# Local attention in ten blocks of 57 queries on a 64x64-split array, in place of five blocks of 120 queries

## The chip, the cores and the metric

One core of one Trainium2 chip. The metric is the device time of one execution in microseconds, the median of three runs. All inputs and outputs are float32.

## The reference

Attention over 4 x 8 heads of 576 positions and 64 columns has two parts: one over positions averaged in fours, one over the neighbours nearer than 4. Their sum goes through two MLPs.

```python
q_d = q.reshape(B, H, Sd, factor, D).mean(axis=3)      # k_d, v_d alike; factor = 4
out_up = np.repeat(sm_attn(q_d, k_d, v_d), factor, axis=2)
mask = np.abs(pos[:, None] - pos[None, :]) < factor
scores = np.where(mask, scale * q @ k.T, -1e9)
out_local = softmax(scores) @ v
x = (out_up + out_local)                               # to 2304 x 512
x = ((x @ w1) * (x @ w2)) @ w3 @ w_out                 # first MLP
h = x @ w_in;  out = (h * sigmoid(h)) @ w_out2         # second MLP
```

## The kernel before

The kernel is written engine by engine: each of the five blocks (`sync`, `gpsimd`, `scalar`, `vector`, `tensor`) is a program of its own, and semaphores with counted values tie them together. Nothing reorders; each engine does what its program says in that order, and a wait holds up all that stands behind it.

Attention takes the heads two at a time, 16 pairs. It is a pipeline of steps `step(i, c, turn, score, weigh, mul, flip)` that `steps` calls in the same way on every engine; the middle twelve are a loop whose body has an odd step (c = 1) and an even one (c = 2). One step turns the next pair's q and k onto channels (`turn`: `turn_in(qn, ...)`, `turn_in(kn, ...)`), computes scores and softmax for this pair (`score`), and for the previous pair turns the probabilities and multiplies them with v (`weigh`). Between these TensorE does a share of the product w3 x w_out (`multiply(0)` to `multiply(3)`, line 905) and turns a piece of w3 for later (`flip`, line 981), which ScalarE copies to `w3t` (`w3_high`) and VectorE completes.

Pooled scores are lines 833 (`qd` by `kd`). Local scores are line 841: five blocks j of 120 queries (`QS`) by 128 keys for each of the two heads side by side, with `kp` holding the keys twice, zero in the other head's channels, so that one product of 128 channels gives both heads. VectorE adds the mask and takes the minimum for each block and head (`mask_local`, line 627; scores carry a minus sign), ScalarE takes ten exponentials with their sums (`exps_local`, line 433), POOL multiplies by the inverse sums (line 359), TensorE turns the probabilities (`turn_p`, line 867), ScalarE copies them to `pt` (`copy_pt`, line 405), TensorE multiplies with v (`weighted`, line 888) and VectorE adds the pooled part into x (`take_local`, line 647). Groups `(0, 1), (2, 3), (4,)` share a PSUM bank. On ScalarE the copies of `pt` and the exponentials of the next pair alternate, and the copies of `w3t` come after the last copy of `pt`:

```python
for j in range(3):
    if weigh:
        copy_pt(2 + j)
    if score:
        exps_local(j)
if flip and weigh:
    w3_high()
```

After the last step TensorE goes through the MLPs in dense loops of products in float32r (line 797), which the change leaves alone.

Of the kernel before, what the change touches and what calls it, by code (L numbers as in the profile page):

```python
# [17 lines left out]
def attention_then_mlps(nc, q, k, v, w1, w2, w3, w_out, w_in, w_out2, out):  # L18
# [24 lines left out]
    NB, QW, KW = 5, 120, 128  # L43
    KS = (S - KW) // (NB - 1)
    QS = [0, 116, 228, 340, 456]
    EW = [b - a for a, b in zip(QS, QS[1:] + [S])]
    MASK_OF = [0, 1, 1, 1, 2]
    assert [a - KS * j for j, a in enumerate(QS)] == [POOL * m for m in MASK_OF]
    GROUPS = [(0, 1), (2, 3), (4,)]
# [9 lines left out]
    with ctx:  # L59
# [3 lines left out]
        def sem(name):  # L63
# [6 lines left out]
        gate_v = sb("gate_v", [1, 6])  # L70
# [9 lines left out]
        vw = sb("vw", [KW, 2, NB, 2 * D], where=att)  # L80
# [4 lines left out]
        kp = sb("kp", [P, 2, 2, S], where=att)  # L85
# [4 lines left out]
            + 2 * S + 4 * S + 3 * SD + 2 * SD + 2 * SD  # L90
# [4 lines left out]
        kd = sb("kd", [P, 2, 2, SD], where=att)  # L95
        mask = sb("mask", [QW, 3, KW], where=att)
        wn = sb("wn", [P, 2, BANK], where=att)
        prob = sb("prob", [QW, 2, NB, 2, KW], where=att)
        prob_d = sb("prob_d", [PD, 2, 2, 2, HS], where=att)
        pt = sb("pt", [KW, NB, 2 * QW], where=att)  # L100
        w3t = sb("w3t", [P, 2, MT, P], F32R, where=att)
        low = sb("low", [QW, 2, 10], where=att)
        lowd = sb("lowd", [PD, 2, 4], where=att)
        lowd16 = sb("lowd16", [PD, 2, 4], where=att)
        tot = sb("tot", [QW, 2, 10], where=att)
        totd = sb("totd", [PD, 2, 4], where=att)
        tot1 = sb("tot1", [QW, 2, 10], where=att)
        totd1 = sb("totd1", [PD, 2, 4], where=att)
        inv = sb("inv", [QW, 2, 10], where=att)
# [36 lines left out]
        qt_ready, kp_ready_a, exp_d, exp_l, pt_ready = (  # L146
            sem("qt_ready"), sem("kp_ready_a"), sem("exp_d"), sem("exp_l"), sem("pt_ready"))

        kp_ready_v, pooled, mind, low_d, masked, x_ready = (
            sem("kp_ready_v"), sem("pooled"), sem("mind"), sem("low_d"), sem("masked"), sem("x_ready"))  # L150
# [42 lines left out]
        def s_bank(c, g):  # L193
            return pS + (5 * c + g) % 2

        def p_bank(g):
            return pP + g % 2
# [5 lines left out]
        def _(sp):  # L203
# [29 lines left out]
            def load_windows(s, u, first):  # L233
                if not first:
                    sp.wait_ge(summed, 4 * (s - 1))
                for j in range(NB):
                    sp.dma_start(vw[:, u, j, :].rearrange("p (h d) -> p h d", h=2),
                                 vf[ds(2 * s, 2), KS * j * D:(KS * j + KW) * D].rearrange(
                                     "h (p d) -> p h d", d=D)).then_inc(v_in[u], 16)
# [168 lines left out]
        def _(act):  # L408
# [9 lines left out]
            def step(i, c, turn, score, weigh, mul, flip):  # L418
# [48 lines left out]
                if score:  # L467
                    exps_down(0)
# [616 lines left out]
```

## Time and profile before

| | |
|---|---|
| median of 3 runs | 920.55 us |
| lowest, highest | 919.85, 921.1 us |
| span of the profiled execution | 918.8 us |
| TensorE, VectorE, ScalarE, POOL busy | 98%, 42%, 35%, 15% of the span |
| granted TensorE clock | 0.9 or more of full in each of 40 slices |
| DMA | 43.5 MB, mean 47 GB/s |

The page gives the profiled execution by its span, from the first instruction to the last; a time of its own for that execution is not listed, and the median of the runs is 1.75 us above the span. Busy shares are means over the whole span. Attention with its softmax work fills roughly the first 217 us, the MLPs the rest.

### The profile page before, as it was taken

Reading aid. Unit: us, or ns where it says so; the run is one execution under the profiler, and the core shown is the slowest. Engines: PE = TensorE matmul, PEld = TensorE weight load, DVE = VectorE, ACT = ScalarE, POOL = GpSimd, SP = SyncE. Lnnn points to the kernel's source line nnn. Section 1 sums busy time; section 2 is a strip of 40 time slices with the busy share of each in tenths; the row PEclk is TensorE's granted clock in tenths of the full one; section 3 lists DMA queues with packets and bytes.
Section 4 is the critical chain, followed back from the end, with each engine's and each line's share of the span. In section 5 each row is a group of like instructions: output and inputs, shape, how many; then the busy total and the mean of one; then the engine's idle time right before and its main releaser. Section 6 shows DMA issues by size and latency. Waiting matters only on the chain.

```text
span 918.8 us, 14849 instructions
## 1 busy us (share of the span) xinstructions
PE 897.4 (98%) x4928; PEld 826.0 (90%) x4928; DVE 382.6 (42%) x1125; ACT 320.3 (35%) x920; POOL 140.8 (15%) x164
## 2 busy tenths in 40 slices
PE   5999999989999999999999999999999999999998
PEld 3888888869999999999999998989898999999997
DVE  6899999985812121212121443231222321322322
ACT  6888888873422221213131322121211211211211
POOL 5744444451800000000003300000000000000000
PEclk9999999999999999999999999999999999999999
DMA  8654444534300000000024200100000000000000
GB/s 213 159 128 121 121 119 120 127 95 118 79 1 1 0 0 0 0 0 1 1 69 130 77 1 1 36 1 0 35 0 0 35 0 0 35 1 1 34 1 35
DMA packets 90567, 43.53 MB, mean 47 GB/s; under 512 B 62112, under 2 KB 83104, under 8 KB 90528
## 3 DMA queue, kind: packets, MB, share of 16 engines
q1 hardware_dynamic: 90528, 43.01, 17.6%
q8 instruction: 24, 0.39, 0.2%
q14 instruction: 15, 0.12, 0.0%
HBM read 38.27 MB, written 4.72 MB: 47 GB/s over the span
## 4 chain that ended last, share of the span: by engine, by line
PE 90%; ACT 4%; DVE 3%; issue 1%; POOL 1%; DMA 0%; ACTq 0%; SPq 0%; DVEq 0%; POOLq 0%
PE ps L797 76%; PE ps L905 3%; PE ps L841 3%; ACT prob L433 2%; PE ps L888 2%; PE ps L822 2%; PE ps L884 1%; PE ps L867 1%; PE ps L833 1%; ACT qt L461 1%; POOL r L345 1%; ACT pt L405 0%; DVE prob L627 0%; DVE r L600 0%; DVE kd L694 0%
## 5 line engine op out<-in xcount | busy, mean ns | idle before, releaser
L797 PE MATMUL ps<-xs,r 128*128 128x384 f32 x2304 | 425.7, 336 | 0.5 <-DVE xs L606 0.5
L797 PEld LDWEIGHTS ps<-xs,r 128*128 128x128 f32 x2304 | 405.1, 188 | 9.2 <-issue 0.9
L797 PE MATMUL ps<-r,gh 128*128 128x512 f32 x576 | 194.8, 392 | 0.0
L572 ACT ACTIVATE gf<-ps 128x384 f32<-128x384 f32 x96 | 47.2, 492 | 320.0 <-PE ps L797 320.0
L764 DVE CAST gh<-gf 128x384 fp32r<-128x384 f32 x96 | 35.0, 365 | 281.6 <-ACT gf L572 281.6
L797 PEld LDWEIGHTS ps<-r,gh 128*128 128x128 f32 x576 | 108.1, 188 | 20.3 <-issue 0.2
L797 PE MATMUL ps<-r,gl 128*128 128x512 f32 x288 | 113.7, 395 | 0.0
L730 DVE TENSOR_TENSOR gf<-ps,osb 128x384 f32<-128x384 f32 x48 | 26.7, 557 | 182.2 <-ACT osb L405 182.2
L405 ACT ACTIVATE osb<-ps 128x384 f32<-128x384 f32 (+1 forms) x60 | 30.8, 514 | 194.1 <-PE ps L797 194.1
L797 PE MATMUL ps<-gh,r 128*128 128x384 f32 x384 | 97.3, 334 | 0.0
L797 PEld LDWEIGHTS ps<-gh,r 128*128 128x128 f32 x384 | 69.3, 188 | 0.0
L433 ACT ACTIVATE prob<-prob,low 120x128 f32<-120x128 f32 x160 | 62.3, 394 | 5.7 <-DVE low L627 5.7
L797 PE MATMUL ps<-gl,r 128*128 128x384 f32 x192 | 64.1, 334 | 0.0
L797 PEld LDWEIGHTS ps<-r,gl 128*128 128x128 f32 x288 | 54.0, 188 | 9.1
L905 PE MATMUL ps<-r,w3t 128*128 128x512 f32 x192 | 56.4, 415 | 1.1 <-DVE r L657 1.1
L766 DVE TENSOR_TENSOR gl<-gf,gh 128x384 fp32r<-128x384 f32 x96 | 54.9, 572 | 3.3
L394 POOL CAST r<-raw 128x512 fp32r<-128x512 f32 x16 | 12.5, 784 | 274.9 <-DMA raw<-in_moe_w_in 274.8
L647 DVE TENSOR_TENSOR x<-ps,od 64x116 f32 (+5 forms) x160 | 43.9, 275 | 11.9 <-issue 5.6
L359 POOL TENSOR_TENSOR prob<-prob,inv 120x1280 f32<-120x1280 f32 x16 | 37.2, 2327 | 74.5 <-DVE inv L670 74.5
L841 PE MATMUL ps<-kp,qt 128*120 128x256 f32 x160 | 40.4, 383 | 0.6 <-DVE low L627 0.6
L733 DVE TENSOR_TENSOR gl<-gf,gh 128x384 fp32r<-128x384 f32 x48 | 28.3, 590 | 28.6 <-ACT gh L405 28.6
L888 PE MATMUL ps<-pt,vw 128*128 128x240 f32 x160 | 37.9, 367 | 0.7 <-ACT pt L405 0.7
(73 smaller groups left out, 858.0 us busy)
## 6 DMA issues: line engine op xcount, KB each, us to landing
raw<-in_moe_w_out SPq DMA_DIRECT2D x24, 256.0 KB, 3.0
vw<-in_v SPq DMA_DIRECT2D x80, 64.0 KB, 2.1
qn<-in_q SPq DMA_DIRECT2D x32, 144.0 KB, 3.0
kn<-in_k SPq DMA_DIRECT2D x32, 144.0 KB, 3.1
out<-osb SPq DMA_DIRECT2D x18, 256.0 KB, 2.1
wn<-in_moe_w SPq DMA_DIRECT2D x16, 256.0 KB, 2.9
raw<-in_moe_w SPq DMA_DIRECT2D x16, 256.0 KB, 4.1
raw<-in_moe_w_in SPq DMA_DIRECT2D x16, 256.0 KB, 4.7
```

Source lines behind the costliest of these rows:

```text
L359: nc.gpsimd.tensor_tensor(pr, pr, inv[:, w, :, None].broadcast_to([QW, 10, KW]), ALU.mult).then_inc(norm_l, 1)
L405: return nc.scalar.activation(o, a, ACT.Copy)
L433: e = nc.scalar.activation(prob[:, u, j, h, :], prob[:, u, j, h, :], ACT.Exp, bias=low[:, u, 2 * j + h:2 * j + h + 1], scale=-1.0, accum_o ...
L572: nc.scalar.activation(gf[:, n % 2, :], ps[:, n % 2, 0:T], ACT.Silu).then_inc(g_ready, 1)
L647: e = nc.vector.tensor_tensor(xf[r, ds(at + QS[j], EW[j])].rearrange("p (t f) -> p t f", f=POOL), ps[r, p_bank(1) if g == 1 else pO, o:o + ...
L733: nc.vector.tensor_tensor(gl[:, n % 2, :], gf[:, n % 2, :], gh[:, n % 2, :].bitcast(F32), ALU.subtract).then_inc(ab_lo, 1)
L764: nc.vector.tensor_copy(gh[:, n % 2, :], gf[:, n % 2, :]).then_inc(g_hi, 1)
L766: nc.vector.tensor_tensor(gl[:, n % 2, :], gf[:, n % 2, :], gh[:, n % 2, :].bitcast(F32), ALU.subtract).then_inc(g_lo, 1)
L797: e = nc.tensor.matmul(o, weights[a][l], tile[a][r], start=(first and a == 0 and p == 0), stop=(last and a == kk - 1 and p == 2))
L841: e = nc.tensor.matmul(ps[0:QW, b, a * 2 * KW:(a + 1) * 2 * KW], qt[:, u, QS[j]:QS[j] + QW], kp[:, u, :, KS * j:KS * j + KW], start=True, ...
L888: e = nc.tensor.matmul(ps[:, b, a * 2 * QW:(a + 1) * 2 * QW], vw[:, w, j, :], pt[:, j, :], start=True, stop=True)
L905: e = nc.tensor.matmul(ps[:, pW, :], w3t[:, l, a, :], r3[:, a, r, :], start=(a == 0 and p == 0), stop=(a == MT - 1 and p == 2))
```

## The change

Local attention is cut into ten blocks of 64 keys instead of five of 128; 57 queries of a block are kept (60 in the first and last). Scores are computed head by head with 64 channels: a product of 64 channels by 64 queries by 64 keys stands on one of four 64x64 tiles of the array, given by the head (which 64 channels) and by the parity of the block (which 64 output partitions). So two blocks lie on 128 partitions, and `prob` is 128 x 5 x 2 x 64 instead of 120 x 5 x 2 x 128. The doubled keys `kp` become plain `kt`, copied by ScalarE alone; the pooled scores, too, are computed head by head with 64 channels. Masking is one operation over all 640 columns, the minimum another; POOL subtracts the minima (a new operation); one exponential covers everything; VectorE sums it. The v windows hold both heads with zeros in the other head's columns, so a weighted sum takes 128 channels (two heads by 64 keys), 128 weight columns and 57 query columns. Three turned groups of probabilities go to one bank and two to the next, and x is taken in two halves of 288 positions. The order on TensorE and ScalarE is written anew.

```diff
-    NB, QW, KW = 5, 120, 128
...
+    BW, NB = 64, 10
+    NG = NB // 2
+    REACH = POOL - 1
+    STEP = BW - 1 - 2 * REACH
+    KS = [STEP * j for j in range(NB - 1)] + [S - BW]
+    OWN = [0] + [STEP * j + REACH for j in range(1, NB)]
+    NQ = [b - a for a, b in zip(OWN, OWN[1:] + [S])]
...
+        def p_place(g):
+            return (pP, 2 * BW * g) if g < LATE else (pP + 1, 2 * BW * (g - LATE))
+        def o_place(half):
+            return (pO, SD) if half == 0 else (pP + 1, 0)
...
+                    pool.wait_ge(min_l, s + 1)
+                    pr = prob[:, u, :, :, :].rearrange("p g h k -> p (g h) k")
+                    nc.gpsimd.tensor_tensor(pr, pr, low[:, u, :, None].broadcast_to([P, 10, BW]), ALU.subtract
+                                            ).then_inc(shifted, 1)
...
+                def exps_local():
+                    act.wait_ge(shifted, s + 1)
+                    pr = prob[:, u, :, :, :].rearrange("p g h k -> p (g h k)")
+                    nc.scalar.activation(pr, pr, ACT.Exp, scale=-1.0).then_inc(exp_l, 1)
...
+                def copy_pt(late):
+                    act.wait_ge(p_turned, 3 * (s - 1) + 2 + late)
+                    act.wait_ge(summed, 3 * (s - 1))
+                    g0, g1 = (LATE, NG) if late else (0, LATE)
+                    b, o = p_place(g0)
+                    copy_act(pt[:, 2 * g0:2 * g1, :].rearrange("p j q -> p (j q)"),
+                             ps[:, b, o:o + (g1 - g0) * 2 * BW]).then_inc(pt_ready, 1)
...
-                for j in range(3):
-                    if weigh:
-                        copy_pt(2 + j)
-                    if score:
-                        exps_local(j)
+                if weigh:
+                    copy_pt(0)
                 if flip and weigh:
                     w3_high()
-                if score:
-                    exps_local(3)
+                if weigh:
+                    copy_pt(1)
...
                 if score:
-                    exps_local(4)
+                    exps_local()
...
+                def mask_local():
+                    dve.wait_ge(scored, 2 * s + 2)
+                    if not weigh:
+                        dve.wait_ge(consts, 5)
+                    nc.vector.tensor_tensor(prob[:, u, :, :, :].rearrange("p g h k -> p h g k"),
+                                            ps[:, pS:pS + 2, 0:NG * BW].rearrange("p h (g k) -> p h g k", g=NG),
+                                            mask[:, None, :, :].broadcast_to([P, 2, NG, BW]), ALU.add
+                                            ).then_inc(masked, 1)
+                    dve.wait_ge(masked, s + 1)
+                    nc.vector.tensor_reduce(low[:, u, :].rearrange("p (g h) -> p g h", h=2), prob[:, u, :, :, :],
+                                            AX.X, ALU.min).then_inc(min_l, 1)
...
+                    dve.wait_ge(exp_l, s)
+                    nc.vector.tensor_reduce(tot[:, w, :].rearrange("p (g h) -> p g h", h=2), prob[:, w, :, :, :],
+                                            AX.X, ALU.add).then_inc(sum_l, 1)
...
-                    else:
-                        if g < 4:
-                            pe.wait_ge(exp_d, 2 * s + g - 1)
-                        else:
-                            pe.wait_ge(masked, 3 * s + 1)
-                        for a, j in enumerate(GROUPS[g - 2]):
-                            e = nc.tensor.matmul(ps[0:QW, b, a * 2 * KW:(a + 1) * 2 * KW],
-                                                 qt[:, u, QS[j]:QS[j] + QW], kp[:, u, :, KS * j:KS * j + KW],
...
+                def scores_down():
+                    pe.wait_ge(pooled, 2 * s + 2)
+                    if c != 0:
+                        pe.wait_ge(masked, s)
+                    for g in range(2):
+                        for h in range(2):
+                            rows = slice(h * D, (h + 1) * D)
+                            e = nc.tensor.matmul(ps[0:PD, pS + h, g * SD:(g + 1) * SD],
+                                                 qd[rows, u, g * PD:(g + 1) * PD], kd[rows, u, :],
...
+                def scores_local():
+                    for g in range(NG):
+                        for h in range(2):
+                            rows = slice(h * D, (h + 1) * D)
+                            for b in range(2):
+                                j = 2 * g + b
+                                e = nc.tensor.matmul(ps[b * BW:(b + 1) * BW, pS + h, g * BW:(g + 1) * BW],
+                                                     qt[rows, u, QS[j]:QS[j] + BW], kt[rows, u, KS[j]:KS[j] + BW],
+                                                     start=True, stop=True)
...
+                def turn_local(late):
+                    if late:
+                        pe.wait_ge(x_ready, 3 * (s - 1))
                     else:
-                        for a, j in enumerate(GROUPS[g - 2]):
-                            for h in range(2):
-                                o = (2 * a + h) * QW
-                                e = nc.tensor.transpose(ps[:, b, o:o + QW], prob[:, w, j, h, :],
-                                                        ident[0:QW, 0:QW])
+                        pe.wait_ge(norm_l, s)
+                        pe.wait_ge(pt_ready, 3 * (s - 1) + 1)
+                    for g in range(LATE, NG) if late else range(LATE):
+                        b, o = p_place(g)
+                        e = nc.tensor.transpose(ps[:, b, o:o + 2 * BW],
+                                                prob[:, w, g, :, :].rearrange("p h k -> p (h k)"), ident[:, :])
...
-                        for a, j in enumerate(GROUPS[g - 1]):
-                            e = nc.tensor.matmul(ps[:, b, a * 2 * QW:(a + 1) * 2 * QW], vw[:, w, j, :],
-                                                 pt[:, j, :], start=True, stop=True)
...
+                def weighted_local(half):
+                    pe.wait_ge(pt_ready, 3 * (s - 1) + 2 + half)
+                    if half == 0:
+                        pe.wait_ge(v_in[w], 16 * 6 * (i + (c - 1) // 2) + 16 * 6)
+                        pe.wait_ge(vw_blank, 2)
+                        pe.wait_ge(x_ready, 3 * (s - 1) + 1)
+                    b, o = o_place(half)
+                    for j in range(NB // 2 * half, NB // 2 * (half + 1)):
+                        at, q0 = o + OWN[j] - half * HALF, OWN[j] - QS[j]
+                        e = nc.tensor.matmul(ps[:, b, at:at + NQ[j]], vw[:, w, j, :], pt[:, j, q0:q0 + NQ[j]],
+                                             start=True, stop=True)
...
-                    scores(2)
-                    scores(3)
-                if weigh:
-                    turn_p(2)
-                    turn_p(3)
+                    pe.wait_ge(exp_d, s + 1)
                 multiply(2)
-                if weigh:
-                    weighted(1)
-                    turn_p(4)
+                if score:
+                    scores_local()
+                if weigh:
+                    turn_local(0)
+                    turn_local(1)
                 multiply(3)
+                if weigh:
+                    weighted_local(0)
                 if flip:
-                    pe.wait_ge(kp_ready_a, s + 2)
-                    pe.wait_ge(kp_ready_v, s + 2)
...
-                if score:
-                    scores(4)
-                if weigh:
-                    weighted(2)
-                    weighted(3)
+                if weigh:
```

TensorE's program, even step of the loop, from the transposes of the probabilities on. `prob` are the probabilities, `r,w3t` the products `multiply`, `pt,vw` the weighted sums, `wn` the w3 transposes, `kp,qt` or `kt,qt` the local scores. Before:

```order
L867 MATMUL ps<-ident,prob 128x120 x8
L905 MATMUL ps<-r,w3t 128x512 x3
L876 REGISTER_ALU
L881 REGISTER_ALU
L888 MATMUL ps<-pt,vw 128x240 x2
L867 MATMUL ps<-ident,prob 128x120 x2
L905 MATMUL ps<-r,w3t 128x512 x3
L981 MATMUL ps<-ident,wn 128x128 x4
L839 ISA
L841 MATMUL ps<-kp,qt 120x256
```

Of the change, the same step from the local scores on:

```order
L854 MATMUL ps<-kt,qt 64x64 x20
L877 MATMUL ps<-ident,prob 128x128 x5
L916 MATMUL ps<-r,w3t 128x512 x3
L891 REGISTER_ALU
L899 MATMUL ps<-pt,vw 128x60
L899 MATMUL ps<-pt,vw 128x57 x4
L984 MATMUL ps<-ident,wn 128x128 x4
L891 REGISTER_ALU
L899 MATMUL ps<-pt,vw 128x57 x4
L899 MATMUL ps<-pt,vw 128x60
```

All local scores now stand together and ahead of the transposes, all probabilities are turned together, and after the w3 transposes nothing stands before the second half of the weighted sums, where a score product stood.

ScalarE's program, even step of the loop, around the copies of `w3t` (the copies of `pt` are turned probabilities, `r<-ps` is the finished product of w3 and w_out). Before:

```order
L405 ACTIVATE pt<-ps 128x240
L431 REGISTER_ALU
L433 ACTIVATE prob,tot<-prob,low 120x128 x2
L494 REGISTER_ALU
L405 ACTIVATE w3t<-ps 128x512
L433 ACTIVATE prob,tot<-prob,low 120x128 x2
L405 ACTIVATE gate_a<-ident 1x1
L405 ISA
L405 ACTIVATE r<-ps 128x512
L431 REGISTER_ALU
L433 ACTIVATE prob,tot<-prob,low 120x128 x2
```

Of the change:

```order
L433 ACTIVATE kt<-ps 128x6x96
L471 REGISTER_ALU
L433 ACTIVATE pt<-ps 128x384
L519 REGISTER_ALU
L433 ACTIVATE w3t<-ps 128x512
L471 REGISTER_ALU
L433 ACTIVATE pt<-ps 128x256
L433 ACTIVATE gate_a<-ident 1x1
L433 ISA
L433 ACTIVATE r<-ps 128x512
L462 ACTIVATE prob<-prob 128x640
```

The last copy of `pt` moved from ahead of `w3t` to behind it, and the exponentials from between the copies to the end of the step.

## Rows read from the trace of the kernel before

**Rows 1.** The page: the span, and TensorE's busy time (share).

```profile
span 918.8 us, 14849 instructions
...
PE 897.4 (98%) x4928; PEld 826.0 (90%) x4928; DVE 382.6 (42%) x1125; ACT 320.3 (35%) x920; POOL 140.8 (15%) x164
```

**Rows 2.** Windows: stretch, length, busy by engine (instructions), granted clock, DMA share.

```profile
core 0: us, PE busy (x) PEld busy (x) DVE busy (x) ACT busy (x) POOL busy (x), PEclk, DMA share, GB/s
...
100.00:140.00 40.00, 39.45 (x250) 33.58 (x249) 36.54 (x161) 32.66 (x119) 20.78 (x27) 1.00 0.51 125
...
220.00:260.00 40.00, 40.00 (x232) 40.00 (x232) 25.08 (x30) 14.85 (x30) 18.80 (x16) 1.00 0.44 112
```

**Rows 3.** Timeline of TensorE, odd step's start and one even step: start, length, operation.

```profile
95.21 0.66 PE L822 MATMUL ps<-ident,qn 96*128 96x96 f32 x6
...
97.78 0.71 PE L822 MATMUL ps<-ident,kn 96*128 96x96 f32 x6 [0.56 <-ACT qt L461]
...
107.60 0.66 PE L822 MATMUL ps<-ident,qn 96*128 96x96 f32 x6
108.09 1.14 PE L833 MATMUL ps<-kd,qd 128*72 128x288 f32 x4
109.07 0.54 PE L861 MATMUL ps<-ident,prob_d 72*112 72x72 f32 x6
109.41 1.64 PE L905 MATMUL ps<-r,w3t 128*128 128x512 f32 x6
110.88 0.66 PE L822 MATMUL ps<-ident,kn 96*128 96x96 f32 x6
111.38 0.93 PE L884 MATMUL ps<-ptd,vd 112*128 112x144 f32 x6
112.14 1.89 PE L841 MATMUL ps<-kp,qt 128*120 128x256 f32 x8
113.88 1.03 PE L867 MATMUL ps<-ident,prob 120*128 120x120 f32 x8
114.67 0.96 PE L905 MATMUL ps<-r,w3t 128*128 128x512 f32 x3
115.47 0.97 PE L888 MATMUL ps<-pt,vw 128*128 128x240 f32 x4
116.28 0.37 PE L867 MATMUL ps<-ident,prob 120*128 120x120 f32 x2
116.41 0.95 PE L905 MATMUL ps<-r,w3t 128*128 128x512 f32 x3
117.20 0.60 PE L981 MATMUL ps<-ident,wn 128*128 128x128 f32 x4
117.64 0.59 PE L841 MATMUL ps<-kp,qt 128*120 128x256 f32 x2
118.07 1.38 PE L888 MATMUL ps<-pt,vw 128*128 128x240 f32 x6
119.28 0.66 PE L822 MATMUL ps<-ident,qn 96*128 96x96 f32 x6
```

**Rows 4.** Groups of weight loads, 97 to 179 us, by shape: busy, mean ns.

```profile
L888 PEld LDWEIGHTS ps<-pt,vw 128*128 128x128 f32 x68 | 12.7, 190 | 1.8 <-issue 0.2
...
L833 PEld LDWEIGHTS ps<-kd,qd 128*72 128x72 f32 x24 | 3.1, 143 | 1.2
```

**Rows 5.** Timeline of ScalarE, the same even step.

```profile
117.00 0.35 ACT L405 ACTIVATE pt<-ps 128x240 f32<-128x240 f32 x1
...
118.02 0.58 ACT L405 ACTIVATE w3t<-ps 128x512 fp32r<-128x512 f32 x1
118.50 0.40 ACT L433 ACTIVATE prob<-prob,low 120x128 f32<-120x128 f32 x1
...
120.60 1.18 ACT L461 ACTIVATE qt<-ps 128x576 f32<-128x576 f32 x1
```

**Rows 6.** Timeline of VectorE, the same step.

```profile
111.26 0.72 DVE L673 TENSOR_REDUCE qd<-qt 128x144 f32<-128x576 f32 x1
```

**Rows 7.** Timeline of POOL, the same step.

```profile
111.42 2.33 POOL L359 TENSOR_TENSOR prob<-prob,inv 120x1280 f32<-120x1280 f32 x1 [5.12 <-DVE inv L670]
...
116.95 1.14 POOL L384 TENSOR_TENSOR prob_d<-prob_d,invd 72x576 f32<-72x576 f32 x1 [0.81 <-DVE invd L703]
```

More of the change, by code:

```diff
@@ L41, in attention_then_mlps @@
     CHUNK_AT = [0, KA, HS + KB]
-    NB, QW, KW = 5, 120, 128
[L44 to L49, printed above, removed]
+    BW, NB = 64, 10
[5 more added lines that the diff above has]
+    NQ = [b - a for a, b in zip(OWN, OWN[1:] + [S])]
+    QS = OWN[:-1] + [S - BW]
+    HALF = S // 2
+    assert OWN[NB // 2] == HALF and max(NQ) <= BW and HALF % POOL == 0
+    assert all(KS[j] <= max(OWN[j] - REACH, 0) and min(OWN[j] + NQ[j] + REACH, S) <= KS[j] + BW for j in range(NB))
+    SHIFT = [a - b for a, b in zip(QS, KS)]
+    assert SHIFT == [0] + [REACH] * (NB - 2) + [0]
     T = 384
@@ L652, in take_local @@
-                    e.then_inc(x_ready, 1)
+                    nc.vector.tensor_tensor(
+                        xf[:, ds(at, HALF)].rearrange("p (t f) -> p t f", f=POOL),
+                        ps[:, b, o:o + HALF].rearrange("p (t f) -> p t f", f=POOL),
+                        od[:, w, half * n:(half + 1) * n, None].broadcast_to([P, n, POOL]), ALU.add
+                    ).then_inc(x_ready, 1)
                 def take_w3o():
@@ L824, in turn_in @@
                     e.then_inc(done, 1)
[L826 to L842 removed]
+                def scores_down():
+                    pe.wait_ge(pooled, 2 * s + 2)
+                    if c != 0:
+                        pe.wait_ge(masked, s)
+                    for g in range(2):
+                        for h in range(2):
+                            rows = slice(h * D, (h + 1) * D)
+                            e = nc.tensor.matmul(ps[0:PD, pS + h, g * SD:(g + 1) * SD],
+                                                 qd[rows, u, g * PD:(g + 1) * PD], kd[rows, u, :],
@@ new lines, in weighted_down @@
+                def weighted_down():
+                    pe.wait_ge(pt_ready, 3 * (s - 1) + 1)
+                    pe.wait_ge(vd_ready, s)
+                    pe.wait_ge(x_ready, 3 * (s - 1))
+                    for a in range(3):
+                        e = nc.tensor.matmul(ps[:, pO, 0:SD], vd[:, w, a, :], ptd[:, a, :],
+                                             start=(a == 0), stop=(a == 2))
+                    e.then_inc(summed, 1)
+                def weighted_local(half):
[4 more added lines that the diff above has]
+                        pe.wait_ge(x_ready, 3 * (s - 1) + 1)
+                    b, o = o_place(half)
+                    for j in range(NB // 2 * half, NB // 2 * (half + 1)):
+                        at, q0 = o + OWN[j] - half * HALF, OWN[j] - QS[j]
+                        e = nc.tensor.matmul(ps[:, b, at:at + NQ[j]], vw[:, w, j, :], pt[:, j, q0:q0 + NQ[j]],
+                                             start=True, stop=True)
```

293 lines of the change are left out of this document (108 added, 185 removed).

## The prediction

> **What bounds the kernel now.** I read the page first: TensorE is busy 98% of the span, but that share averages different stages [rows 1]. The stretches divide them. From 100 to 140 us, inside attention, TensorE is busy 39.45 of 40 us, VectorE 36.54 and ScalarE 32.66. From 220 us, in the MLPs, TensorE is busy all the time and nothing of the change is left [rows 2]. So the change works only before about 217 us, and there the question is how long one attention step keeps TensorE.
>
> Next the timeline of TensorE through one step [rows 3]. A matmul's record is longer than the time it keeps the array, so I take differences of starts. An even step (the second of the loop body) runs from its q transposes at 107.60 to the next ones at 119.28: 11.68 us with no idle time. The odd step before The odd step before it runs from 95.21 to 107.60: 12.39 us.. The difference is the k transposes at 97.78, which waited 0.56 us for ScalarE's copy of q. The mean is 12.03 us. In the even step the parts are: pooled scores 0.98, local scores 1.74 + 0.43 = 2.17, probability transposes 0.79 + 0.13 = 0.92, weighted sums of the local part 0.81 + 1.21 = 2.02. The other 5.59 stay.
>
> What does a matmul cost? Eight float32 matmul records with 256 columns take 1.74 us (217 ns each), four with 288 take 0.98 (245), six with 144 take 0.76 (127), six transposes with 96 take 0.50 (83): 0.83 ns a column and some 4 ns, two records for each float32 matmul of the program, one for each transpose. The weight loads lie underneath. Their lengths grow too [rows 4]: 143 ns for 72 columns, 190 for 128. That is 0.84 ns a column on a base of 83, so a load of 128 columns keeps its path for about 107 ns, hidden now behind passes of 120 to 217 ns.
>
> **The change part by part.**
>
> Local weighted sums: 20 passes of 57 to 60 columns instead of 10 of 240. By columns they take 20 x 0.052 = 1.05 us. But each pass still needs a load of 128 columns, 107 ns. Lower bound 1.05, upper bound load and pass one after the other, 20 x 0.157 = 3.1. I take loads overlapped with passes and themselves the bound, since the 144-column row (127 ns a pass) shows overlap down to nearly this size: 20 x 0.11 = 2.2. So 40% of the columns saves nothing: +0.18.
>
> Local scores: 40 passes of 64 columns on four tiles of 64x64. One after the other: 40 x 0.057 = 2.3, plus nothing for loads of 64 columns (53 ns). If neighbouring tiles overlap, the second pass of one matmul runs beside the first of the next: 21 slots x 0.057 = 1.2. If all four tiles ran freely, about 0.6. If loads never hide, 4.4. I take 1.2: -0.97.
>
> Pooled scores: 8 passes of 144 columns, 0.98 in a row as now, five slots = 0.6 with two row tiles overlapped. I take 0.6: -0.38 in an even step. In an odd step the k transposes stand right behind and wait for ScalarE's copy of q. That chain is the drain of q's last transpose with a signal 0.2, the copy 1.18 [rows 5], a signal 0.06: 1.44 us. It is longer than 0.6 + 0.34 + switches, so the odd step goes from 2.07 (97.78 less 95.21 less the 0.50 of the transposes) to 1.44: -0.63 whatever the tiles do below 1.1. ScalarE is free in time for it since its exponentials shrink, below.
>
> Probability transposes: 5 of 128 columns at the 0.11 of the four at 117.20: 0.55, so -0.37.
>
> Switches of the array's shape: the step goes from whole array to 64-row tiles and back, then to 64x64 and back, four times. No row of before has one. Bounds: 0, and 0.16 each (the four at 117.20 have a record of 0.60 and keep the array 0.44, so 0.16 is what drains). I take 0.1: +0.4 in an even step; in an odd one two lie in ScalarE's chain, +0.2. The Trainium skill, TensorEngine Tiling (Array Packing), Key Properties, says that changing the tiling mode, unlike changing the tile, drains the engine; no run here shows it yet. By that rule with the 0.16 the sum would be 0.2 us a step worse, without a drain 0.3 better.
>
> A new wait. ScalarE's order is now copy of the first half of pt, both copies of w3t in place, then the second half of pt; TensorE's is w3 transposes, then the weighted sums that need that half. Before, all pt copies stood ahead of w3t. So after the last w3 transpose TensorE waits: drain and signal 0.2, w3t 0.48 (118.02 to 118.50), pt of 256 columns 0.36, signal 0.05 [rows 5]: 1.1 us in every step that transposes w3. Queued behind it are the second weighted sums and the next step. +1.1.
>
> Softmax. ScalarE drops ten exponentials of about 0.40 for one of 640 columns (0.7, from the 512-column rows). VectorE drops ten masked minima, its half of the k copy and half of kd's reduction; it gains one sum, and a mask and a minimum over 640 columns, about 0.8 each from its 0.72 for 576 [rows 6]. POOL's normalisation of 1280 elements at 2.33 halves, and its new subtraction costs the same half [rows 7]. All three end far under 11 us a step. Since they do not bound, this is worth only the 0.56 wait counted above. The chain local scores, mask 0.8, minimum 0.8, POOL 1.2, exponential 0.7, with signals about 4.0 us, has 5.6 us until the q copy needs ScalarE: hidden with 1.6 to spare. DMA moves the same bytes of v in the same 256-byte pieces.
>
> Sum. Odd: -0.63 - 0.97 - 0.37 + 0.18 + 0.2 + 1.1 = -0.49. Even: -0.38 - 0.97 - 0.37 + 0.18 + 0.4 + 1.1 = -0.04. Mean -0.27. Thirteen steps transpose w3 while weighing: -3.5. The last two have no such wait: without it a step gains 1.1 more than the mean, 1.4, but VectorE and ScalarE split the first layer's weights there, so I take -2 together instead of -2.8. The first two, bound by chains and not by TensorE, gain one POOL operation of 1.2 in front of another: +1. Total -4.5 on the profiled span of 918.8; 1.75 us lie between that span and the median 920.55. **916.0 us.**
>
> **The rivals.**
>
> (a) Tiles do not overlap, slower. Local scores 2.3 and pooled 0.98: odd +0.68, even +1.44, mean 1.06 x 13 + 1 = **935**. For it: each pass is only 57 ns, no shorter than the shortest pair of load and pass in the trace (six transposes of 72 columns in 0.34). It decides from local scores above 1.6. The same skill page, Instruction Overhead, warns against taking the factor from a dimension that is already small, which is what blocks of 64 columns do; no run here shows it.
>
> (b) Half-way: local scores 1.75, pooled 0.8: odd +0.05, even +0.71, 0.38 x 13 - 1 + 1 = **925.5**.
>
> (c) The loads of 128 columns do not bind: 1.05 instead of 2.2 takes 1.15 from each of 16 steps: **898**. For it: no row shows a load as the bound. Against it: lengths that grow with columns exactly.
>
> (d) The softmax chain takes the place of the array: if POOL's subtraction takes over 2.8 instead of 1.2 us, each further tenth comes on every step; at 3.5 us that is 0.7 x 14 = **926**. Against it: POOL's two rows agree at 1.8 and 2.0 ns an element.
>
> (e) The change does what it says but the wide operations free TensorE of more than I see: only 0.56 us in odd steps is idle, so this has no room and no chance of its own.
>
> **How the numbers follow.** Forecast 0.31 (909 to 918.5), (c) 0.22 (892 to 909), (b) 0.20 (918.5 to 930), (a) 0.22 (930 to 941), (d) 0.05. About 0.2% is what a measurement of this kernel can tell from no change. Faster: 0.31 less a little, plus (c): 0.51. Same: the seam between the forecast and (b): 0.10. Slower 0.39. The range leaves out the far half of (a) and of (c): 897 to 936. The forecast's own is 909 to 918.5.
>
> **What the profile after would show.** TensorE's step period: 11.9 odd, 11.6 even. Local scores, from first start to the next line: 1.2 (forecast), 2.3 (a). Weighted sums: two runs of 1.1, (c) 0.5. A wait of TensorE on pt by ScalarE of about 1.1 after the w3 transposes. Gaps of 0.1 at the shape's changes. The granted clock stays 1.00 as in [rows 2], its 2.4 GHz level, since the waits stay as short as the 1.4 us above. VectorE and ScalarE 60% busy between 100 and 140 us. The prediction is wrong if the tiles neither overlap nor hide their loads, or if drains cost several tenths each.

## The result, and the profile after

The change takes 935.65 us (median of 4 runs, 933.34 to 937.09) beside 920.83 us of the kernel before on the same chip (919.85 to 922.71): a ratio of 1.016, 95% interval 1.0139 to 1.018. It is slower by 1.6%. The forecast was 916.0.

The page of the changed kernel, beside [rows 1]: the span, busy times, the granted clock in 40 slices, and the chain of work that ended last.

```profile
span 935.3 us, 14947 instructions
...
PE 894.0 (96%) x5552; PEld 824.0 (88%) x5552; DVE 333.4 (36%) x630; ACT 263.1 (28%) x584; POOL 145.0 (16%) x186
...
PEclk9889888898999999999999999999999999999999
...
PE 81%; SPq 12%; issue 2%; DVE 2%; DMA 1%; POOL 1%; ACT 0%; ACTq 0%; DVEq 0%; POOLq 0%
```

Two things are new. SPq, the time in which SyncE issues DMAs, ends 12% of the span; in the chain of before it had no per cent. And the clock is 0.8 in seven slices of the first ten, where before had 0.9 or more everywhere. TensorE's busy time is hardly lower (894.0 us against 897.4); an operation at half the clock takes longer, as the q transposes below show.

Windows of the changed kernel (stretch, length, busy by engine with counts, granted clock, DMA share, GB/s). The second answers to the first row of [rows 2]; the third and fourth are single steps.

```profile
60.00:100.00 40.00, 35.47 (x355) 29.50 (x353) 26.14 (x50) 19.89 (x50) 18.75 (x26) 0.91 0.46 114
...
100.00:140.00 40.00, 34.67 (x328) 28.97 (x329) 22.60 (x44) 19.29 (x49) 16.13 (x23) 0.83 0.46 114
...
103.53:117.03 13.50, 12.53 (x113) 10.54 (x114) 7.27 (x14) 6.29 (x15) 5.82 (x8) 0.80 0.53 129
...
157.67:169.19 11.52, 10.28 (x115) 8.56 (x115) 8.31 (x16) 6.16 (x15) 5.82 (x8) 1.00 0.43 104
```

VectorE fell from 36.54 to 22.60 us of 40 and ScalarE from 32.66 to 19.29, as foreseen, and TensorE now idles 5.3 of 40 us. The two single steps have the same instructions, and differ in the granted clock: 13.50 us at 0.80, 11.52 at 1.00. The timeline of TensorE through the step from 103.53 and into the next shows both losses, and the wait that was foreseen (start, length, operation, idle time ahead of it):

```profile
100.34 1.32 PE L899 MATMUL ps<-pt,vw 128*128 128x57 f32 x10 [0.96 <-ACT pt L433]
103.53 1.22 PE L832 MATMUL ps<-ident,qn 96*128 96x96 f32 x6 [1.87 <-DMA qn<-in_q]
...
115.87 1.32 PE L899 MATMUL ps<-pt,vw 128*128 128x57 f32 x10 [0.96 <-ACT pt L433]
117.03 0.67 PE L832 MATMUL ps<-ident,qn 96*128 96x96 f32 x6
```

At 103.53 TensorE waited 1.87 us for q to land; before, the steps in [rows 3] begin without a wait. The six transposes behind it took 1.22 us, and those at the next step's start 0.67: the earlier six ran at a granted clock of 0.50, TensorE's 1.2 GHz level, the later ones at 1.00, 2.4 GHz. Of the thirteen steps that begin between 39 and 196 us, five begin with such a wait, of 0.75 to 2.87 us.

Why q is late stands in SyncE's timeline. Its issues in one step of the changed kernel (those of k and w3 left out):

```profile
99.61 1.45 SPq L225 DMA_DIRECT2D qn<-in_q  x2
...
102.62 2.07 SPq L244 DMA_DIRECT2D vg<-in_v  x4
...
105.54 2.51 SPq L254 DMA_DIRECT2D vw<-in_v  x2
108.23 0.52 SPq L257 DMA_DIRECT2D vw<-in_v  x1
108.94 2.23 SPq L254 DMA_DIRECT2D vw<-in_v  x2
111.36 0.50 SPq L257 DMA_DIRECT2D vw<-in_v  x1
112.07 1.39 SPq L225 DMA_DIRECT2D qn<-in_q  x2
```

and of the kernel before:

```profile
107.79 2.62 SPq L237 DMA_DIRECT2D vw<-in_v  x5
...
111.05 1.37 SPq L210 DMA_DIRECT2D qn<-in_q  x2
```

The v windows hold SyncE from 105.54 to 111.86, 6.3 us; before they held it 2.6. From q to q it issues without a pause for 112.07 - 99.61 = 12.46 us, more than a step of TensorE's work now takes. The waits of SyncE between 60 and 200 us, before and after (us in total, times, longest), say the same as slack:

```profile
SPq L237 <- PE ps L888: 30.3, 12, 6.8
SPq L229 <- POOL vt L366: 12.9, 10, 1.8
```

```profile
SPq L254 <- PE ps L899: 2.2, 2, 1.4
```

Before, SyncE waited some 2.5 us in each step until TensorE had finished with the old windows, and about 1.1 more for POOL: 3.6 us of slack. The windows' loading grew by 3.7. Now it is TensorE that waits. The transfers of q themselves are no slower: from issue to landing they take 2.9 us (median) in the changed kernel and 3.0 before, so q is late because it is issued late.

By step starts: from the start that stands at 47.12 before (52.61 after) to the one at 179.75 (195.06 after) lie eleven steps, 132.63 us before and 142.45 after. So 5.5 us are lost before the first of these starts and 9.8 in the eleven steps; the other 1.2 of the 16.5 us between the two profiled spans (935.3 and 918.8) are lost behind them.

### The profile page after: what moved, and what is told of

It reads as the page before. It is cut to its first block, busy times and chain, and to the rows that moved or that the text cites. A ratio compares the mean times of both kernels' runs of the same rounds, so it can differ in the third digit from the quotient of the medians.

```text
span 935.3 us, 14947 instructions
## 1 busy us (share of the span) xinstructions
PE 894.0 (96%) x5552; PEld 824.0 (88%) x5552; DVE 333.4 (36%) x630; ACT 263.1 (28%) x584; POOL 145.0 (16%) x186
## 4 chain that ended last, share of the span: by engine, by line
PE 81%; SPq 12%; issue 2%; DVE 2%; DMA 1%; POOL 1%; ACT 0%; ACTq 0%; DVEq 0%; POOLq 0%
PE ps L807 73%; SPq L254 5%; PE ps L916 3%; SPq L244 2%; SPq L225 2%; PE ps L899 1%; SPq L233 1%; SPq L257 1%; DVE r L622 1%; PE ps L832 1%; PE ps L886 1%; DMA qn<-in_q 1%; DMA vg<-in_v 1%; PE ps L866 1%; DVE xs L628 1%
## 5 line engine op out<-in xcount | busy, mean ns | idle before, releaser
L916 PE MATMUL ps<-r,w3t 128*128 128x512 f32 x192 | 66.8, 478 | 0.3 <-DVE r L676 0.3
L899 PEld LDWEIGHTS ps<-pt,vw 128*128 128x128 f32 x320 | 39.3, 193 | 19.3 <-ACT pt L433 16.8
L899 PE MATMUL ps<-pt,vw 128*128 128x57 f32 (+1 forms) x320 | 41.4, 278 | 13.5 <-ACT pt L433 13.5
L916 PEld LDWEIGHTS ps<-r,w3t 128*128 128x128 f32 x192 | 40.2, 230 | 6.5 <-issue 0.4
L807 PEld LDWEIGHTS ps<-gl,r 128*128 128x128 f32 x192 | 36.0, 188 | 0.0
L433 ACT ACTIVATE gh<-gf 128x384 fp32r<-128x384 f32 x48 | 25.2, 526 | 36.4 <-DVE gf L740 36.4
```

The lines of the kernel that those rows point to most:

```text
L433: return nc.scalar.activation(o, a, ACT.Copy)
L807: e = nc.tensor.matmul(o, weights[a][l], tile[a][r], start=(first and a == 0 and p == 0), stop=(last and a == kk - 1 and p == 2))
L899: e = nc.tensor.matmul(ps[:, b, at:at + NQ[j]], vw[:, w, j, :], pt[:, j, q0:q0 + NQ[j]], start=True, stop=True)
L916: e = nc.tensor.matmul(ps[:, pW, :], w3t[:, l, a, :], r3[:, a, r, :], start=(a == 0 and p == 0), stop=(a == MT - 1 and p == 2))
```

## The experiments

### The windows' loading, the wait on pt, and how much is the array's

Two theories. **Queue theory**: the array gains what was forecast or more, and SyncE's issuing of the v windows takes it back. **Array theory**: the 64-row and 64x64 tiles, their switches and the 128-column loads cost more than forecast. Four kernels.

`v_once` is the changed kernel with the 57-row transfers issued only for the first two pairs. Later pairs work on the old v, so it leaves out that loading:

```diff
-                    for r0, r1 in ((0, STEP), (STEP, BW)):
+                    for r0, r1 in ((0, STEP), (STEP, BW))[0 if isinstance(s, int) and s < 2 else 1:]:
...
-                        pe.wait_ge(v_in[w], 16 * 6 * (i + (c - 1) // 2) + 16 * 6)
+                        pe.wait_ge(v_in[w], 16 * 4 * (i + (c - 1) // 2) + 16 * 6)
```

> The changed kernel, but the two large v transfers of a step (57 rows by 9 blocks) are issued only for the first two pairs; later pairs use the old v, so this leaves out loading. Queue theory (SyncE's queue, 6.3 us a step on v windows against 2.6 before, sets the step at 12.9 us and starves TensorE of q): SyncE has time to spare, no wait of TensorE on q, step falls to TensorE's own 11.4 to 11.6, time 909 to 915. Array theory (the step is set by TensorE's own work plus its 1 us wait on the last copy of pt): nothing changes, 933 to 937.

Measured: 926.45 us (8 runs), ratio 1.0046 [1.0026, 1.0066].

Between 60 and 200 us TensorE has no wait on q in it, and SyncE waits 37.9 us on TensorE.

`before_sp` is the kernel before with the change's four transfers of v, per step, into a buffer that nobody reads:

```diff
+                for h in range(2):
+                    for r0, r1 in ((0, 57), (57, 64)):
+                        sp.dma_start((spare0, spare1)[u][h * 64 + r0:h * 64 + r1, :, :],
+                                     vf[ds(2 * s + h, 1), r0 * D:(r0 + 9 * 57) * D].rearrange(
+                                         "o (j p d) -> p (o j) d", j=9, d=D)[0:r1 - r0]).then_inc(v_in[u], 16)
```

> The kernel before, with four more v transfers a step of the changed kernel's shapes (two of 57 rows by 9 blocks, two of 7 by 9) into an unused buffer; the array's work is untouched. Queue theory: SyncE's step grows from 8.1 by some 5.3 to 13.2 us or more, TensorE waits for q and the time is 935 to 945. Array theory: SyncE waited on TensorE before, the transfers fit into that, 920 to 923.

Measured: 947.59 us (4 runs), ratio 1.0269 [1.0245, 1.0292], 2.6 us above the range of the queue theory.

`split48` cuts the windows at row 48 in place of 57. The bytes, the 256-byte pieces and the number of transfers stay:

```diff
-                    for r0, r1 in ((0, STEP), (STEP, BW)):
+                    for r0, r1 in ((0, 48), (48, BW)):
```

> The changed kernel with the v windows split at row 48 instead of 57, so rows 48 and 16 by 9 blocks; same bytes, 576 pieces of 256 B either way for a head. If issue time follows the pieces: 576 at 4.1 ns a piece, same 6.3 us a step, 933 to 937. If it is the odd row count 57 that is dear (q has 576 pieces in 0.6 us with 96 rows): v windows 3.5 us or less a step, SyncE has time to spare, 909 to 915. Array theory: no change either way.

Measured: 923.92 us (7 runs), ratio 1.0027 [1.0012, 1.0042].

`pt_first` moves ScalarE's copy of the second half of pt ahead of w3t:

```diff
                 if weigh:
                     copy_pt(0)
-                if flip and weigh:
-                    w3_high()
                 if weigh:
                     copy_pt(1)
+                if flip and weigh:
+                    w3_high()
```

> The changed kernel with ScalarE's second copy of pt ahead of the copies of w3t. Queue theory: the 1 us wait of TensorE goes, but only moves into the wait on q, 932 to 937. Array theory: 13 steps lose 1.0 us each, 920 to 924.

Measured: 933.1 us (4 runs), ratio 1.0114 [1.0096, 1.0132].

The queue theory stands for the wait on q, though not, as will be seen, for the whole of the time. Into a kernel whose array work is untouched, the same transfers alone brought 2.7%, part of it again by the clock (0.985 to 0.989 over the whole of its runs, 0.994 to 1.000 in the kernel before); q still took 3.0 us from issue to landing. SyncE in `before_sp`, and TensorE's wait for that q:

```profile
99.14 2.62 SPq L239 DMA_DIRECT2D vw<-in_v  x5
101.86 4.75 SPq L244 DMA_DIRECT2D spare<-in_v  x4
107.33 1.40 SPq L212 DMA_DIRECT2D qn<-in_q  x2
```

```profile
111.52 0.71 PE L829 MATMUL ps<-ident,qn 96*128 96x96 f32 x6 [1.02 <-DMA qn<-in_q]
```

And cutting at another row took 11.7 us off the change. SyncE in `split48`, its timeline and then its wait on TensorE between 60 and 200 us:

```profile
109.57 0.86 SPq L254 DMA_DIRECT2D vw<-in_v  x2
...
111.22 1.05 SPq L254 DMA_DIRECT2D vw<-in_v  x2
```

```profile
SPq L254 <- PE ps L899: 32.7, 12, 7.8
```

The pair of transfers takes 0.86 to 1.05 us in place of 2.23 to 2.51, and SyncE has its slack back, 32.7 us.

`pt_first` shows what a removed wait is worth while another bound stands behind it. The 0.96 us on pt are gone, and the step from 91.31 is still 12.99 us long, because TensorE waits the longer for q:

```profile
100.07 1.22 PE L899 MATMUL ps<-pt,vw 128*128 128x57 f32 x10
104.30 1.22 PE L832 MATMUL ps<-ident,qn 96*128 96x96 f32 x6 [3.01 <-DMA qn<-in_q]
```

But `v_once` and `split48`, 909 to 915 by the queue theory, came out 11 and 9 us above that range. Steps of `split48`, windows:

```profile
84.07:97.85 13.78, 12.82 (x115) 10.67 (x115) 7.73 (x15) 6.93 (x17) 5.81 (x8) 0.78 0.43 107
97.85:109.37 11.52, 10.28 (x115) 8.56 (x115) 8.32 (x16) 6.17 (x15) 5.82 (x8) 1.00 0.51 128
109.37:120.36 10.99, 10.03 (x115) 8.55 (x115) 7.72 (x15) 6.78 (x17) 5.82 (x8) 1.00 0.48 118
```

At clock 1.00 the steps take 11.52 and 10.99 us, no more than the 11.4 to 11.6 expected. But the step at 84.07 is of the second kind, has the same instructions as the step at 109.37 and no wait more, and takes 2.8 us longer at 0.78. From 49.69 to 180.11 eleven steps took 130.42 us, where six of 11.52 and five of 10.99 make 124.07: 6.4 us go to lower clock.

### The remaining wait, and the clock

Two theories of the clock. **Idle theory**: it falls because TensorE idles about a microsecond in every step, and stays up once the pt wait is gone. **Wait-only theory**: the wait costs its own length, and no more. `both` is `split48` with `pt_first`. `flip_early` is `split48` with the w3 transposes moved, in TensorE's program, ahead of the first half of the weighted sums, so that ScalarE has both copies done sooner; `both_early` has all three edits.

```diff
-                if weigh:
-                    weighted_local(0)
                 if flip:
...
+                if weigh:
+                    weighted_local(0)
```

> The changed kernel with the v windows split at row 48 and with the second copy of pt ahead of the copies of w3t. Idle theory (in the split-48 kernel the wait of 0.96 us on pt costs itself and also lets the granted clock fall to half in some steps, 2.8 us each, six or so of sixteen): the wait goes, granted clock stays 0.98 or above through attention, step 10.2 to 10.8, time 896 to 904. Wait-only theory (the clock falls for another reason, say the many small matmuls): only 13 times 1.0 us, 909 to 912, granted clock still 0.83 to 0.97 in 40 us stretches.

> The changed kernel with the v windows split at row 48 and, on TensorE, the w3 transposes ahead of the first weighted sums instead of between the halves; ScalarE's order is as in the change. TensorE now has 1.05 us of weighted sums to do while ScalarE copies w3t and pt. Idle theory: the wait shrinks to nothing, granted clock 0.98 or above, 896 to 904. Wait-only theory: 909 to 912 with drops of the clock.

> Both reorderings and the split at row 48. If a wait for w3t (ScalarE's copy, then VectorE's) remains in the kernel with pt first, as the 0.2 to 1 us seen before the q transposes suggests, this one is 1 to 3 us faster than it: 894 to 902. If not, the same within 1 us.

Measured: `both` 908.29 us (4 runs), ratio 0.9856 [0.9842, 0.987]; `flip_early` 912.28 (4 runs), 0.9909 [0.9892, 0.9927]; `both_early` 912.21 (6 runs, 909.09 to 918.02), 0.9897 [0.9874, 0.992]. All three beat the kernel before. `both` lies between its two ranges, `flip_early` at the upper end of the wait-only range, and `both_early` 10 us above its own. In `both` the clock is 1.00 from 60 to 180 us, as the idle theory has it. What is left stands in the middle of the q transposes, and VectorE's timeline beside it says why:

```profile
123.82 1.22 PE L899 MATMUL ps<-pt,vw 128*128 128x57 f32 x10
124.88 0.42 PE L832 MATMUL ps<-ident,qn 96*128 96x96 f32 x3
125.88 0.47 PE L832 MATMUL ps<-ident,qn 96*128 96x96 f32 x3 [0.58 <-DVE w3t L725]
```

```profile
123.32 0.85 DVE L714 TENSOR_SCALAR totd<-totd 72x4 f32<-72x4 f32 x1
...
124.77 0.46 DVE L667 TENSOR_TENSOR x<-ps,od 128x288 f32 x1 [0.39 <-issue]
125.14 0.68 DVE L725 TENSOR_TENSOR w3t<-ps,w3t 128x512 fp32r<-128x512 f32 x1
```

The last three q transposes go to the bank in which the w3 pieces still lie. VectorE empties it last, with L725, and stands behind the addition into x and a `totd` of four columns that takes 0.85 us.

`both_early` contradicts the idle theory. Its longest wait between 60 and 180 us is that of 0.6 us, as in `both`, yet the step from 91.93 to 105.67 took 13.74 us at clock 0.75, where the one from 70.20 to 81.28, with the same instructions and wait, took 11.08 at 1.00. (The profiled execution, 918.02, was its slowest.) The wait-only theory falls too, since `both` gained more than the wait's length. The kernels with shorter waits mostly kept a higher clock; whether the waits are the cause, and what makes the clock fall in one step and not in another, these runs don't tell.

### Do tiles run at once?

`same_tile` is `both` with the forty score passes in another order: all ten of one tile, then the next tile's.

```diff
-                    for g in range(NG):
-                        for h in range(2):
-                            rows = slice(h * D, (h + 1) * D)
-                            for b in range(2):
+                    for h in range(2):
+                        rows = slice(h * D, (h + 1) * D)
+                        for b in range(2):
+                            for g in range(NG):
```

> As the kernel with split at row 48 and pt first, but the twenty local score matmuls ordered tile by tile (five in a row on each 64x64 tile) instead of going round the tiles. In the changed kernel 40 passes of 64 columns take 0.74 us, 18 ns a pass where one pass alone needs 53 by its columns. If the overlap of tiles makes that, tile by tile takes 2.1 to 2.3 us. If a pass of 64 columns is just short, 0.74 again.

Measured: 926.63 us (one run), 18 above `both`. The scores in `same_tile`, and in `split48` in the change's order:

```profile
119.08 2.00 PE L854 MATMUL ps<-kt,qt 64*64 64x64 f32 x40
121.01 0.77 PE L877 MATMUL ps<-ident,prob 128*128 128x128 f32 x5
```

```profile
100.45 1.63 PE L916 MATMUL ps<-r,w3t 128*128 128x512 f32 x6
101.92 0.90 PE L886 MATMUL ps<-ptd,vd 112*128 112x144 f32 x6
102.56 0.96 PE L916 MATMUL ps<-r,w3t 128*128 128x512 f32 x3
103.45 0.81 PE L854 MATMUL ps<-kt,qt 64*64 64x64 f32 x40
104.19 0.77 PE L877 MATMUL ps<-ident,prob 128*128 128x128 f32 x5
...
106.64 0.61 PE L984 MATMUL ps<-ident,wn 128*128 128x128 f32 x4
108.21 1.32 PE L899 MATMUL ps<-pt,vw 128*128 128x57 f32 x10 [0.96 <-ACT pt L433]
109.37 0.67 PE L832 MATMUL ps<-ident,qn 96*128 96x96 f32 x6
```

By starts, 1.93 us tile by tile (48 ns a pass) and 0.74 in turn (18.5 ns): going round the tiles gains a factor of 2.6, and work on different tiles overlaps. Whether it is the passes, their weight loads or both, no run separates, nor was the order of the PSUM banks, which changes with the order of the tiles, varied by itself. Sixteen pairs at 1.19 us are 19.0, about the whole difference of the times. A shape switch is read in the same rows. Three products of 512 columns keep the array 0.74 us (half of the six from 100.45 to 101.92) to 0.80 (104.71 to 105.51), and the scores start 0.89 after the three of 102.56 do: 0.09 to 0.15 us for the switch.

### VectorE's order

`both_dve` is `both` with VectorE's L725 ahead of the addition into x. `early_dve` is `both_early` with it ahead of `totd` as well:

```diff
-                if score:
-                    dve.wait_ge(exp_d, s + 1)
-                    nc.vector.tensor_scalar(totd1[:, u, :], totd[:, u, :], 1e-9, float(POOL), ALU.add,
...
-                if weigh:
-                    take_local(0)
...
+                if score:
+                    dve.wait_ge(exp_d, s + 1)
...
+                if weigh:
+                    take_local(0)
```

> As the kernel with the split at row 48 and pt first, and VectorE finishes w3t before it takes the first half of x, instead of after. There TensorE stopped 0.6 us in each step ahead of the last three q transposes for this w3t. If VectorE's order makes that wait: shorter by 0.3 to 0.4 us a step (one operation of 0.38), 13 steps, 903 to 905. If ScalarE's copy decides it: no change, 907 to 909.

> The split at row 48, pt first, w3 transposes ahead of both weighted sums, and VectorE finishes w3t before the pooled sums' reciprocal. The wait on w3t should be gone: 0.6 us by 13 steps less than the kernel with split and pt first, 899 to 902, if the granted clock stays as high; if it falls as it did in the earlier kernel with the early transposes (0.979 against 0.992), 903 to 908.

Measured: `both_dve` 903.48 us (5 runs), ratio 0.9796 [0.9777, 0.9815]; `early_dve` 898.23 us (5 runs, 895.61 to 899.66), ratio 0.9747 [0.973, 0.9764]: the first as expected if VectorE's order makes the wait, the second 0.8 us under its range. The latter is the fastest kernel of this study: 22.8 us under the kernel before and 37.4 under the change, with the change's own arithmetic. Its step is free of waits from weighted sums to the next q:

```profile
115.05 2.34 PE L899 MATMUL ps<-pt,vw 128*128 128x60 f32 x20
117.22 0.67 PE L832 MATMUL ps<-ident,qn 96*128 96x96 f32 x6
...
127.04 0.67 PE L832 MATMUL ps<-ident,qn 96*128 96x96 f32 x6
```

The step from 117.22 takes 9.82 us, and eleven steps from 46.77 to 157.36 a mean of 10.05.

### Why 57 rows are dear

`split48` left open what in 57 rows costs so much. `split53` and `split56` are `split48` with the cut at row 53 and at row 56.

> The change with its v windows cut into rows 0 to 53 and 53 to 64 in place of 57 and 7 (same bytes, same 256-byte pieces, same number of transfers). Known from the runs so far: SyncE issues 57 rows and 7 rows of nine pieces in 2.1 us together, 48 and 16 rows in 0.85. Two theories of why. Divisor theory: the price goes with the number of pieces over the largest divisor of the row count that is at most 16 (57 rows: 513 pieces over 3 = 171; 48 rows: 432 over 16 = 27; 7 rows: 63 over 7 = 9). From the two pairs: 2.1 = 2a + 180b and 0.85 = 2a + 36b (16 rows: 9), so b = 8.7 ns and a = 0.27 us. 53 is prime: 477 over 1, and 11 rows: 99 over 11 = 9, so 0.54 + 486 x 0.0087 = 4.8 us for the pair. SyncE's step grows by 2 x 2.7 = 5.4 us on 12.5, and the time by about 15 x 5.2 on 935.65: 1014 us, between 990 and 1035. Piece theory: odd or large row counts are dear by their number of pieces alone: 477 pieces cost what 513 do, the pair 2.0 us, and the time stays at 930 to 938. The Trainium skill, DMA: Bandwidth & Descriptors, section on why a DMA increments its semaphore by 16, says that a transfer runs on as many DMA engines as the largest number up to 16 that divides its slowest dimension; it gives no price for the issue.

> The change with its v windows cut into rows 0 to 56 and 56 to 64: one row fewer than the change's 57. Divisor theory: 56 rows have the divisor 14, 504 pieces over 14 = 36, and 8 rows 72 over 8 = 9: 0.54 + 45 x 0.0087 = 0.93 us for the pair in place of 2.1, SyncE's step 10.1 us, TensorE no longer waits for q, and the time is split48's, 921 to 927. Piece theory: 504 pieces cost what 513 do, 2.1 us the pair, and the time is that of the change, 933 to 938.

Measured, one run each: `split53` 1059.28 us, `split56` 923.55 us, with 919.71 for the kernel before beside them. SyncE in `split53`, then in `split56`:

```profile
151.11 6.61 SPq L254 DMA_DIRECT2D vw<-in_v  x2
```

```profile
111.37 0.97 SPq L254 DMA_DIRECT2D vw<-in_v  x2
```

One row fewer than 57 makes the pair 0.97 us in place of 2.2; four rows fewer make it 6.6. So the number of pieces alone does not set the price (477 against 513), and the piece theory falls; the four cuts come in the order that the divisor theory gives. The divisor theory sized the dear end too low: 6.4 to 7.5 us where it expected 4.8, and 1059 where it expected 1014, outside the range given. From 53 rows the price is nearer 13 ns for each piece of the largest share than the 8.7 worked out from 57 and 48, so it isn't one straight line.

## Why the prediction was wrong

**The step that failed** is the last sentence of the softmax paragraph: "DMA moves the same bytes of v in the same 256-byte pieces". The sentence is true of bytes and pieces, and the term was priced at nothing without a look at the queue. What changed was SyncE's time to issue the transfers, and [rows 1 to 7] hold no row of SyncE. The kernel before would have shown a queue with 3.6 us of slack a step; the change adds 3.7, and by the forecast TensorE's step was to get 0.27 shorter. Two runs show it from both sides: `before_sp` (2.7% slower by the transfers alone) and `split48` (the same change, 1.3% faster than the change by one number). `split53` and `split56` show that the price goes with the row count. The Trainium skill, DMA: Bandwidth & Descriptors, in the section on why a DMA increments its semaphore by 16, has the rule that would have warned: a transfer runs on as many DMA engines as the largest number up to 16 that divides its slowest dimension, so by it 57 rows go to 3 and 48 to 16. The four cuts (48, 53, 56, 57) fall in the order of that rule; no row here names the engines of one transfer.

**"The granted clock stays 1.00"** was wrong too: 0.91, then 0.83 in the two stretches above. The argument, that waits no longer than 1.4 us do nothing, came from a kernel that waits once in two steps. `split48`, with the queue mended, still lost 6.4 of 130 us to it.

**How the loss divides.** In the eleven steps the change took 142.45 us and `split48` 130.42: the cut at row 57 costs 12.0. Only 4.7 of these are TensorE's waits for q (four of them, 0.75 to 1.87 us); the other 7.3 are steps at a lower clock. `split48`'s 130.42 against 124.07 at full clock: 6.4 more for clock. So some 14 us of the eleven steps are clock, three times what the waits for q cost by their own length, and the forecast had neither. And 124.07 against the forecast's 11 x 11.76 = 129.4: 5.3 better than forecast. Before the loop the change lost 5.5 us where +1 was given; `split48` begins its steps 2.6 us later than before (49.69 against 47.12), so 2.9 of them came with the cut at row 57.

**The terms of the sum**, from the rows of `split48` at full clock:
- Local scores: forecast 1.2, measured 0.74, mis-sized. The sum took two neighbouring tiles at a time, and the overlap is greater. With `same_tile`'s 1.93 this speaks against rival (a), which had 2.3, and against (b).
- Pooled scores: forecast 0.6, measured 109.97 to 110.61, 0.64. Right.
- Transposes of probabilities: forecast 0.55, measured 104.19 to 104.71, 0.52. Right.
- Weighted sums: forecast 2.2, measured 1.13 (105.51 to 106.64) and 1.16 (108.21 to 109.37), 2.29. Right in size, and (c), with 1.05 for both, is out. A pass of 57 columns takes 105 to 116 ns, beside the 107 worked out for the load of 128 columns; that the load is the bound fits these numbers, but no run varied it.
- The new wait: forecast 1.1; the array is free at about 106.64 + 0.44 = 107.08 and goes on at 108.21, 1.13. Right. Removing it gained little in the change (`pt_first`: 2.5 us by the times, 4 by the ratios), and 15.6 us once the queue was mended (`both` against `split48`). That is not 13 x 1.13: ten steps of `both` take 108.72 us against 118.89, and of these 10.2 us only 3.9 are at full clock (10.87 a step against 11.26), since the wait on VectorE's w3t took the place of the rest; 6.3 are clock.
- Switches: forecast 0.1 each, measured 0.09 to 0.15, and 0.10 from q's transposes to the pooled scores (97.85 to 98.45, less the 0.50 of the transposes). Right for these two; the two switches back lie inside the 0.64 and 0.74 above and could not be read by themselves. The Trainium skill, TensorEngine Tiling (Array Packing), Key Properties, has a drain at each change of mode, and the gaps of about 0.1 us agree with it.
- Steps: forecast 11.9 and 11.6, measured 11.52 and 10.99.
- Softmax: VectorE is 56% busy and ScalarE 48% between 100 and 140 us of the change, 73% and 66% in the faster steps of `early_dve` (29.08 and 26.26 of 40), where 60% were forecast; POOL's subtraction 1.26 us where 1.2 was forecast. Rival (d) needed 2.8 and is out.

The time, 935.65, lies at rival (a)'s 935, but (a) said that tiles do not overlap, and they do. That agreement is chance: a right sum by a wrong mechanism would have sent an engineer to the score order, where there was nothing to mend. That the same skill page, Instruction Overhead, advises against a tiling factor from a dimension that is already small was what I weighed for (a); here, forty passes of 64 columns were 2.6 times faster in turn round the four tiles than tile by tile, so for this shape the measurement decides against the rule.

## What to carry to other kernels

A changed transfer has three prices: bytes, pieces, and the time its queue takes to issue it. Ask first how much slack the issuing queue has in a step, and cut transfers at row counts that a number near 16 divides (here 48 and 56, which 16 and 14 divide, were cheap to issue; 57 and 53, with 3 and 1, were dear). When several waits stand one behind another, removing one shows its worth only after the one behind it is gone: the wait on pt was worth 2.5 us (4 by the ratios) before the queue was mended and 15.6 after, more than its own length, since less low clock came with it. When a change makes an engine's work lighter, look again at the order of its small operations; here another cut of the windows and four small moves on ScalarE, TensorE and VectorE turned a change that cost 1.6% into one that saves 2.5%.

## What was not expected of the hardware

- Issue time by row count, two transfers of nine 256-byte pieces a row: 48 + 16 rows 0.85 to 1.1 us, 56 + 8 rows 0.8 to 1.0, 57 + 7 rows mostly 2.1 to 2.5, 53 + 11 rows 6.4 to 7.5.
- Forty passes of 64x64x64 on four tiles in turn take 18.5 ns each, and 48 ns each on one tile at a time.
- The clock falls in kernels whose longest wait in a step is about 1 us, and even at 0.6 (`both_early`); the deepest of these steps lost 2.7 to 3.1 us. In `split53`, with waits for q of 7.5 us on average between 20 and 330 us, it was 0.6 or 0.7 in most of the first 13 slices.
- VectorE's `totd`, four columns, took 0.85 us at 123.32 in `both` and 0.16 in `early_dve`. POOL's timeline in `both`, then VectorE's in `early_dve`:

```profile
122.89 1.26 POOL L408 TENSOR_TENSOR prob<-prob,low 128x640 f32<-128x640 f32 x1 [1.07 <-DVE low L652]
```

```profile
116.48 0.16 DVE L723 TENSOR_SCALAR totd<-totd 72x4 f32<-72x4 f32 x1
```

In `both`, `totd` begins inside POOL's new subtraction and ends at 124.17, just behind its end at 124.15; in `early_dve` the subtraction runs from 115.27 to 116.53 and `totd` begins as it ends. The Trainium skill, SBUF — State Buffer, section SBUF: two separate sides, says that VectorE and GpSimd share a pair of ports as an exclusive lock, held for a whole instruction, which on VectorE's side concerns operations in a mode that uses both ports and those with two inputs in SBUF; in which mode `totd` ran, no row shows. The rows agree with it; no run took the subtraction away to show it by itself.
